# The last seven tiles' rows of the first layer made inside the first route; their logits from the squared relus

## The chip, the cores and the metric

The kernel runs on one core of a Trainium2 chip. The metric is the device time of the whole program in microseconds (us). The engines are TensorE (PE; its weight loads are listed as PEld), VectorE (DVE), ScalarE (ACT), GpSimd (POOL) and SyncE (SP), which here only issues DMAs.

## The reference, cut to what matters

Bucketed attention over 2 x 8 heads of 768 tokens gives `x` (1536 tokens, 512 columns). A dense layer follows, and then a second layer that sends each token to one of eight experts:

```python
def _moe_ref(x, w_in, w_out):
    h = np.maximum(x @ w_in, 0.0)
    return (h * h @ w_out).astype(np.float32)

def _moe2_ref(x, w_gate, w1, w2):
    logits = x @ w_gate
    order = np.argsort(-logits.flatten())
    # in this order a token takes an expert, if it has none and the expert
    # has fewer than N // E = 192 tokens
    ...
    for e in range(E):
        mask = assigned == e
        h = np.maximum(x[mask] @ w1[e], 0.0)
        out[mask] = h @ w2[e]
```

The assignment needs the logits of all 1536 tokens before the first expert can start.

## The kernel before

Three stages follow one another: attention, the first layer (`first_layer`), and `experts`, which also holds the routing.

**The first layer** takes the tokens in `CHUNKS` = 4 chunks of `HALF` = 384 tokens. For each chunk it goes through `FT` = 16 tiles of 128 hidden units. Products are made from 32-bit operands split in a high part (a rounded copy) and a low part (the rest). For a tile `f` of a chunk:

- PE, `hidden` (L946): 12 products of 384 columns into bank `PB[f % 2]`.
- ACT, `tile`: the relu out of the bank (L952), its square as high part `h_hi` (L954), then `in_high` (L963), the high part of the `w_in` tile two tiles on, and `out_high` (L966), that of the next `w_out` tile.
- DVE, `hidden`: the square in 32 bits (L1143) and its rest `h_lo` (L1146).
- POOL, `both_low`: the low parts of the `w_in` tile (L970) and of the `w_out` tile (L974). `hidden` two tiles on waits for the first (`wils`).
- PE, `rows` (L1227): 9 products of 512 columns (three token tiles by hi-hi, hi-lo, lo-hi), which add this tile's part to the 384 rows in banks `PB[2]` to `PB[4]`.

PE runs one tile ahead: `hidden(f + 1)`, then `rows(f)`. The order on each engine is the order of the code; semaphores join the engines. During the next chunk's first tiles, ACT copies the rows out, SP stores them to `y_rows` in DRAM, PE turns them (`turn`, L1241) and multiplies them with `w_gate` (`logits`, L1249). Behind the fourth chunk no tile is left to do this beside: ACT copies (L1135), PE turns (L1302) and multiplies (L1310), DVE and ACT copy between them, and a barrier between the two code blocks (L1864) ends the stage.

**The routing** finds which tokens an expert gets. `choose` (DVE, from L1537) takes each token's best expert; `route` goes through five digit levels (`LEVELS`). In each level DVE compares (L1561), PE counts with 12 products of 8 columns (L1719), DVE looks which experts fill (L1569), PE sums (L1721), DVE takes the digit. Then come three more steps (L1725; L1687 and L1688; L1694), the last of which makes the list of tokens. ACT copies the list (L1465), POOL gathers those rows from `y_rows` by an indirect DMA (L1427), PE turns them (L1741) and the expert starts (L1776, L1790). The later routes run between products of the experts; for the first there are none. `keep_warm` (L1799) issues idle products of 512 columns there, five behind each of its steps 10 and 11, and more in the steps of the second route.

SP loads the first half of the first expert's `w1` (L1409) when the route has named the expert.

## Time and profile before

| | us |
|---|---|
| median of 3 runs | 799.44 (798.57 to 799.66) |
| the profiled execution, its own time | 798.89 |
| its span, first to last instruction | 797.2 |
| PE busy | 771.8 (97%) |
| DVE busy | 368.7 (46%) |
| ACT busy | 378.6 (47%) |
| POOL busy | 400.0 (50%) |

The span is what the profile sees of the profiled execution; 1.69 us of its time lie outside. Busy time counts an engine's instructions; since the records of matmuls overlap, a stream's cost is read from start to start and not from the durations.

### The profile page before, as it was taken

How to read it: one execution, taken by the hardware profiler on the slowest of the kernel's cores; microseconds unless marked ns; L12 is line 12 of the kernel's file. 1: busy time of each engine (PE TensorE's matmuls, PEld its weight loads, DVE VectorE, ACT ScalarE, POOL GpSimd, SP SyncE). 2: the span in 40 equal slices, each digit the busy share in tenths (PEclk: the TensorE clock that was granted, in tenths of full speed). 3: DMA queues.
4: the chain of work that ended last, by engine and by line, in shares of the span. 5: the costliest groups of instructions: out<-in, count | busy, mean ns of one | idle time of the engine just before them, and what ended most of it. 6: DMA issues, size and time to landing. Idle time of an engine off the chain costs nothing. (4 is left out here: it accounts for less than half of the span.)

```text
span 797.2 us, 13826 instructions
## 1 busy us (share of the span) xinstructions
PE 771.8 (97%) x4620; PEld 700.2 (88%) x4622; DVE 368.7 (46%) x854; ACT 378.6 (47%) x664; POOL 400.0 (50%) x326
## 2 busy tenths in 40 slices
PE   7999999999999999999999999996799999999996
PEld 6898889889978888999999999995399999999996
DVE  7576576666754454232242225224654554454000
ACT  3677767767677655535555554552021222122221
POOL 5677777777686786656555666562100120011101
PEclk9999999999999999999999999998599999999999
DMA  7675776665554000000010001001264743654741
GB/s 161 145 175 134 154 163 161 144 160 133 128 114 137 0 1 0 14 28 0 0 39 0 0 0 41 0 0 40 74 230 161 249 148 133 224 190 164 263 136 40
DMA packets 44220, 81.44 MB, mean 102 GB/s; under 512 B 17192, under 2 KB 17192, under 8 KB 43664
## 3 DMA queue, kind: packets, MB, share of 16 engines
q1 hardware_dynamic: 41968, 74.58, 33.3%
q0 software_dynamic: 2048, 6.29, 2.4%
q8 instruction: 25, 0.41, 0.2%
q14 instruction: 19, 0.16, 0.1%
q10 hardware_dynamic: 160, 0.00, 0.0%
HBM read 54.55 MB, written 6.29 MB: 76 GB/s over the span
## 5 line engine op out<-in xcount | busy, mean ns | idle before, releaser
L312 POOL TENSOR_TENSOR pt_lo<-pt,pt_hi 128x768 fp32r<-128x768 f32 x64 | 117.8, 1846 | 51.2 <-ACT pt_hi L449 43.8
L946 PE MATMUL banks<-xt_hi,split_parts 128*128 128x384 f32 (+1 forms) x512 | 141.3, 337 | 0.5 <-POOL split_parts L970 0.5
L970 POOL TENSOR_TENSOR split_parts<-w_in_sb,split_parts 128x512 fp32r<-128x512 f32 x64 | 85.0, 1329 | 85.4 <-ACT split_parts L963 84.1
L1143 DVE TENSOR_TENSOR h<-relu 128x384 f32<-128x384 f32 x64 | 43.0, 671 | 177.2 <-ACT relu L952 177.1
L1227 PE MATMUL banks<-split_parts,h_hi 128*128 128x512 f32 x384 | 120.6, 395 | 0.2
L442 ACT ACTIVATE pt<-banks 128x768 f32<-128x768 f32 x96 | 78.1, 813 | 65.3 <-PE banks L719 55.0
L563 DVE TENSOR_REDUCE mx<-banks 128x1 f32<-128x768 f32 x96 | 90.5, 957 | 22.8 <-PE banks L747 18.7
L946 PEld LDWEIGHTS banks<-xt_hi,split_parts 128*128 128x128 f32 x512 | 93.5, 188 | 3.5 <-issue 0.9
L1776 PE MATMUL banks<-x_cols,w_in_sb 128*128 128x192 f32 x512 | 92.6, 333 | 0.4 <-ACT x_cols L1471 0.4
L1790 PE MATMUL banks<-expert_hidden,w_out_sb 128*128 128x192 f32 x512 | 92.2, 332 | 0.0
L974 POOL TENSOR_TENSOR split_parts<-w_out_sb,split_parts 128x512 fp32r<-128x512 f32 x64 | 84.5, 1320 | 13.7 <-ACT split_parts L966 13.7
L946 PE MATMUL banks<-xt_lo,split_parts 128*128 128x384 f32 (+1 forms) x256 | 86.1, 336 | 0.0
L1776 PEld LDWEIGHTS banks<-x_cols,w_in_sb 128*128 128x128 f32 x512 | 82.4, 191 | 2.4 <-issue 0.8
L1790 PEld LDWEIGHTS banks<-expert_hidden,w_out_sb 128*128 128x128 f32 x512 | 83.2, 191 | 0.6
L1227 PEld LDWEIGHTS banks<-split_parts,h_hi 128*128 128x128 f32 x384 | 70.4, 188 | 13.3 <-DVE h_lo L1146 1.4
L1434 POOL DMA_INDIRECT out<-expert_out,rows_of_out x14 | 13.2, 946 | 135.6 <-ACT expert_out L1486 133.5
L1227 PE MATMUL banks<-split_parts,h_lo 128*128 128x512 f32 x192 | 75.9, 395 | 0.0
L952 ACT ACTIVATE relu<-banks 128x384 f32<-128x384 f32 x64 | 31.5, 492 | 86.5 <-PE banks L946 86.5
L718 PE MATMUL banks<-qa,ka 128*128 128x384 f32 x190 | 68.7, 362 | 0.8 <-ACT pt L442 0.7
L719 PE MATMUL banks<-qb,kb 128*128 128x384 f32 x190 | 63.8, 336 | 0.0
L966 ACT ACTIVATE split_parts<-w_out_sb 128x512 fp32r (+1 forms) x64 | 40.6, 634 | 41.0 <-PE banks L1227 41.0
L1494 ACT ACTIVATE expert_hidden<-banks 128x192 f32<-128x192 f32 x64 | 21.2, 332 | 71.7 <-PE banks L1776 71.7
(239 smaller groups left out, 1329.8 us busy)
## 6 DMA issues: line engine op xcount, KB each, us to landing
w_out_sb<-in_moe_w SPq DMA_DIRECT2D x8, 2048.0 KB, 8.4
w_in_sb<-in_moe_w SPq DMA_DIRECT2D x7, 2048.0 KB
w_in_sb<-in_moe_w_in SPq DMA_DIRECT2D x8, 512.0 KB, 6.9
w_out_sb<-in_moe_w_out SPq DMA_DIRECT2D x8, 512.0 KB, 5.7
w_out_sb<-in_k SPq DMA_DIRECT2D x16, 192.0 KB, 3.9
w_out_sb<-in_q SPq DMA_DIRECT2D x16, 192.0 KB, 4.0
v_raw<-in_v SPq DMA_DIRECT2D x16, 192.0 KB, 3.7
ka<-split_parts SPq DMA_DIRECT2D x16, 192.0 KB, 3.0
```

Of the source, the lines that this page charges most:

```text
L312: pool.tensor_tensor(pt_lo[x % 2][:], pt[j % 2][:], pt_hi[x % 2][:].bitcast(fp32), ALU.subtract).then_inc(los, 1)
L442: act.activation(halves(pt[j % 2]), both(ST), ACT.Exp, scale=SCALE).then_inc(ex, 1)
L563: dve.tensor_reduce(mx[:, j:j + 1], both((PREP, SM)[j % 2]), AX.XY, ALU.max).then_inc(mxs, 1)
L718: pe.matmul(ST[:, h, 0:HALF], ka[i][:, kc], qa[i][:, c], start=True, stop=False)
L719: last = pe.matmul(ST[:, h, 0:HALF], kb[i][:, kc], qb[i][:, c], start=False, stop=True)
L946: last = pe.matmul(PB[i][:, 0:HALF], w_[:, k, :], x_[:, xs], start=n == 0, stop=n == 3 * DT - 1)
L970: pool.tensor_tensor(wil[i], in_view(f), wih[i].bitcast(fp32), ALU.subtract).then_inc(wils, 1)
L974: pool.tensor_tensor(wol[i], out_view(f), woh[i].bitcast(fp32), ALU.subtract).then_inc(wols, 1)
L1143: dve.tensor_tensor(h32[i][:], r32[i][:], r32[i][:], ALU.mult)
L1227: last = pe.matmul(PB[2 + t][:], h_[:, tc], w_[:], start=start and n == 0, stop=stop and n == 2, skip_group_check=True)
L1776: last = pe.matmul(PB[2 + f % 2][:, 0:CAP], w1s[i][:, k, f * P:(f + 1) * P], xgt[:, k, :], start=k == 0, stop=k == DT - 1)
L1790: last = pe.matmul(PB[4 + d % 2][:, 0:CAP], w2s[i][:, f, d * P:(d + 1) * P], hs[:, f, :], start=f == 0, stop=f == F2T - 1)
```

## The change

- The fourth chunk keeps its 16 `hidden` steps, but makes the `rows` products of its first `F0` = 9 tiles only. The squared relus of tiles 9 to 15 and the split parts of their `w_out` tiles are kept (`kept`, `late_parts`), most of them in space that the attention's result no longer needs. The `w_out` parts are made during the third chunk: on every second tile from tile 3 on ACT makes one high part more and POOL one low part more (7 each).
- The 63 products left out (3 token tiles x 7 hidden tiles x 3) go to `late_rows`: 6 behind the last `hidden`, 57 between the steps of the first route (`FILL`), where the ten `keep_warm` products go.
- The fourth chunk's logits are a sum of two. The rows of tiles 0 to 8 are copied out (`part`), turned (`part_turn`) and multiplied (`part_logits`, 16 columns wide, half of them zeros) beside the last `hidden` steps. For tiles 9 to 15 the logits come from the squared relus times `wogs`, which is `w_out` times `w_gate` in a high and a low part: `gate_sums_of`, two products of 384 columns for each of tiles 9 to 14, and `last_logits` for tile 15, which also turns those sums (3 products) and adds all up in `PB[6]`. It runs behind the barrier; DVE adds the halves by one reduction (L1868 of the new kernel).
- `w_out` times `w_gate` for the seven tiles is made by DVE during the first three chunks: 56 times `tensor_tensor_reduce` over 128x512 (three after a tile in chunk 0, two in chunks 1 and 2). SP loads the columns of `w_gate` as eight rows on all partitions (a further input `gate_rows`), and ACT copies each row to PSUM (8 copies), from where DVE reads it.
- DVE's square reads the relu's bank beside the relu (`scalar_tensor_tensor`) and no longer the relu twice. `hidden` of tile g waits for `h_lo` of tile g - 2 in place of its relu.
- The fourth chunk's rows are stored in three DMAs, each behind one ACT copy in `experts`; the DVE's wait for the stores in level 1 of the first route goes, POOL's wait before the first gather stays. On SP the three stores stand ahead of the load of `w1`.
- Constants of the routing (DVE, POOL) are made one or two a tile in the fourth chunk and not in one go.

The core of the diff:

```diff
+F0 = 9
+REST = FT - F0
+LATE_PARTS = {3: 9, 5: 10, 7: 11, 9: 12, 11: 13, 13: 14, 15: 15}
+PRODUCTS = 3 * CT * REST
+AHEAD = 6
+FILL = (14, 1, 6, 1, 5, 1, 5, 1, 5, 1, 4, 12, PRODUCTS)
...
+    def late_rows(pe, first, last):
+        for x in range(first, min(last, PRODUCTS)):
+            t, r = divmod(x, 3 * REST)
+            f, n = divmod(r, 3)
+            f += F0
...
+            h_, w_ = ((h_hi, w_hi), (h_hi, w_lo), (h_lo, w_hi))[n]
+            done = pe.matmul(PB[2 + t][:], h_[:, t * P:(t + 1) * P], w_, start=False, stop=r == 3 * REST - 1, skip_group_check=True)
+            if r == 3 * REST - 1:
+                done.then_inc(row_tile, 1)
...
         def _(dve):
-                dve.tensor_tensor(h32[i][:], r32[i][:], r32[i][:], ALU.mult)
+                dve.scalar_tensor_tensor(h32[i][:], PB[i][:, 0:HALF], 0.0, r32[i][:], ALU.max, ALU.mult)
...
+            def gate_part(c, x):
+                n, d = divmod(x, REST)
+                e = GATES * c + n
...
+                dve.tensor_tensor_reduce(made[:], wo[:, (F0 + d) * DM:(F0 + d + 1) * DM], PB[5 + n][:], 1.0, 0.0, ALU.mult, ALU.add,
+                                         wog[:, d, e:e + 1])
...
             def hidden(g, x0, i):
-                pe.wait_ge(relus, g - 1)
+                pe.wait_ge(hls, g - 1)
                 split["hidden"](pe, g, x0, i)
...
+            def gate_sums_of(f):
...
+                pe.wait_ge(hls, last_g + f + 1)
+                for n, h_ in enumerate(kept(f)):
+                    last = pe.matmul(PB[7][0:2 * E, P:P + HALF], wogs[:, f - F0, :], h_, start=f == F0 and n == 0, stop=f == FT - 2 and n == 1)
...
+            def last_chunk(x0):
+                c = CHUNKS - 1
+                for f in range(FT):
+                    g, i = last_g + f, f % 2
+                    if f + 1 < FT:
+                        hidden(g + 1, x0, 1 - i)
+                    else:
+                        late_rows(pe, 0, AHEAD)
...
+                    elif f == F0 + 1:
+                        part_turn(0)
+                    elif f == F0 + 2:
+                        part_turn(1)
+                    elif f == F0 + 3:
+                        part_logits(0)
+                        part_turn(2)
+                    elif f == F0 + 4:
+                        part_logits(1)
+                    elif f == F0 + 5:
+                        part_logits(2)
+                    if f < F0:
+                        rows(g, i, f == 0, False)
+                    elif f < FT - 1:
+                        gate_sums_of(f)
...
         def _(sp):
+            for t in range(CT):
+                sp.wait_ge(y_tile, t + 1)
+                at = (CHUNKS - 1) * HALF + t * P
+                sp.dma_start(y_rows[at:at + P, :], last_rows[t]).then_inc(stored, 16)
...
-            pool.wait_ge(stored, 16 * CHUNKS)
             pool.memset(oh[:, CH:P], 0.0).then_inc(padded, 1)
+            pool.wait_ge(stored, STORED)
...
-                    if l == 1 and not past(s, 1):
-                        dve.wait_ge(stored, 16 * CHUNKS)
...
+            dve.wait_ge(logit, 1)
+            dve.tensor_reduce(L[:, NT - CT:NT, :], PB[6][:, 0:2 * E * CT].rearrange("p (t a e) -> p t e a", t=CT, a=2), AX.X, ALU.add)
...
-            for k in range(STEPS):
+            last_logits(pe).then_inc(logit, 1)
+            at = AHEAD
+            for k, fill in enumerate(FILL):
+                late_rows(pe, at, at + fill)
+                at += fill
                 routing(0, k)
-                if 2 * NL <= k < STEPS - 1:
+                if k >= 2 * NL and at >= PRODUCTS and k < STEPS - 1:
                     keep_warm(5)
```

**PE in the fourth chunk, around one of its later tiles.** Before, a tile's `rows` (L1227) stand behind each `hidden` (L946):

```order
L946 MATMUL banks0<-xt_lo,split_parts 128x384
L946 MATMUL banks0<-xt_hi,split_parts 128x384
L1227 MATMUL banks1<-split_parts,h_hi1 128x512 x2
L1227 MATMUL banks1<-split_parts,h_lo1 128x512
L1227 MATMUL banks1<-split_parts,h_hi1 128x512 x2
L1227 MATMUL banks1<-split_parts,h_lo1 128x512
L1227 MATMUL banks2<-split_parts,h_hi1 128x512 x2
L1227 MATMUL banks2<-split_parts,h_lo1 128x512
```

Now (L958 is `hidden`, L1401 `part_logits`, L1392 `part_turn`, L1410 `gate_sums_of`), between `hidden` of tile 13 and of tile 14:

```order
L958 MATMUL banks0<-xt_hi,split_parts 128x384 x2
L958 MATMUL banks0<-xt_lo,split_parts 128x384
L958 MATMUL banks0<-xt_hi,split_parts 128x384
L1401 MATMUL banks3<-w_gate_and_zeros,y_t0 128x16 x4
L1392 MATMUL banks2<-ident,turned 128x128 x4
L1410 MATMUL banks3<-xt_hi,gate_of_hidden_parts 16x384
L1410 MATMUL banks3<-xt_lo,gate_of_hidden_parts 16x384
L958 MATMUL banks0<-xt_hi,split_parts 128x384
```

The nine products of 512 columns have gone from here; two of 384 columns and the small ones of the logits have come.

**PE from the last hidden tile to the first route.** Before: the last rows, the turned rows (L1302), the logits (L1310), the two blocks' branches, and the route's counting:

```order
L1227 MATMUL banks2<-split_parts,h_hi1 128x512 x2
L1227 MATMUL banks2<-split_parts,h_lo1 128x512
L1302 MATMUL banks2<-ident,y_rows_sb 128x128 x4
L1302 MATMUL banks3<-ident,y_rows_sb 128x128 x4
L1302 MATMUL banks0<-ident,y_rows_sb 128x128 x4
L1310 MATMUL banks3<-w_gate_sb,y_t0 128x8 x4
L1310 MATMUL banks3<-w_gate_sb,y_t1 128x8 x4
L1310 MATMUL banks3<-w_gate_sb,y_t2 128x8 x4
L1864 UNCONDITIONAL_BRANCH
L1683 UNCONDITIONAL_BRANCH
L1719 MATMUL banks3<-chosen16,reaches 128x8 x12
L1721 MATMUL banks3<-fills,level_weights 128x8
```

Now: the last `gate_sums_of`, six late products (L1026), the branches, and `last_logits` (L1498, L1503):

```order
L1410 MATMUL banks3<-h_hi0,gate_of_hidden_parts 16x384
L1410 MATMUL banks3<-h_lo0,gate_of_hidden_parts 16x384
L1026 MATMUL banks1<-xt_hi 128x512
L1026 MATMUL banks1<-xt_lo,xt_hi 128x512
L1026 MATMUL banks1<-xt_hi,xt_lo 128x512
L1026 MATMUL banks1<-xt_hi 128x512
L1026 MATMUL banks1<-xt_lo,xt_hi 128x512
L1026 MATMUL banks1<-xt_hi,xt_lo 128x512
L2070 UNCONDITIONAL_BRANCH
L1882 UNCONDITIONAL_BRANCH
L1498 MATMUL banks3<-ident,relu0 128x16 x3
L1503 MATMUL banks3<-gate_of_hidden_parts,h_hi1 128x16
```

Turns and logits of the rows stand ahead of the barrier, in the run of hidden tiles; what is left behind the branches is `last_logits` and the late products after it.

**PE in the digit levels of the first route.** Before, nothing stands between its steps until L1799:

```order
L1719 MATMUL banks3<-chosen16,reaches 128x8 x12
L1721 MATMUL banks3<-fills,level_weights 128x8
L1719 MATMUL banks3<-chosen16,reaches 128x8 x12
L1721 MATMUL banks3<-fills,level_weights 128x8
L1725 MATMUL banks3<-chosen_counts,ones16 128x192
L1799 MATMUL banks1<-level_table0,level_weights 128x512 x5
L1687 MATMUL banks3<-members_up_to_tile,ones16 128x24
```

Now, two levels (L1918 counts, L1920 sums, L1026 are late products):

```order
L1918 MATMUL banks3<-chosen16,reaches 128x8 x12
L1026 MATMUL banks1<-xt_hi 128x512
L1920 MATMUL banks3<-fills,level_weights 128x8
L1026 MATMUL banks1<-xt_lo,xt_hi 128x512
L1026 MATMUL banks1<-xt_hi,xt_lo 128x512
L1026 MATMUL banks1<-xt_hi 128x512
L1026 MATMUL banks1<-xt_lo,xt_hi 128x512
L1026 MATMUL banks1<-xt_hi,xt_lo 128x512
L1918 MATMUL banks3<-chosen16,reaches 128x8 x12
L1026 MATMUL banks1<-xt_hi 128x512
L1920 MATMUL banks3<-fills,level_weights 128x8
```

Each counting step has five products of 512 columns ahead of it, each summing step one.

**DVE in the first three chunks.** Before, a tile is its two operations:

```order
L1143 TENSOR_TENSOR h0<-relu0 128x384
L1146 TENSOR_TENSOR h_lo0<-h0,h_hi0 128x384
L1142 REGISTER_ALU
L1143 TENSOR_TENSOR h1<-relu1 128x384
L1146 TENSOR_TENSOR h_lo1<-h1,h_hi1 128x384
```

Now, in chunk 1 (L1262 is the new reduction, with a short second instruction for its sum):

```order
L1246 SCALAR_TENSOR_TENSOR h0<-banks0,relu0 128x384
L1249 TENSOR_TENSOR h_lo0<-h0,h_hi0 128x384
L1262 ISA gate_products,gate_of_hidden<-w_out_sb,banks3 128x512
L1262 ISA gate_of_hidden 128x1
L1262 ISA gate_products,gate_of_hidden<-w_out_sb,banks3 128x512
L1262 ISA gate_of_hidden 128x1
L1246 SCALAR_TENSOR_TENSOR h1<-banks0,relu1 128x384
L1249 TENSOR_TENSOR h_lo1<-h1,h_hi1 128x384
```

Two reductions that read PSUM stand behind each tile's pair.

## Rows read from the trace of the kernel before

**Rows 1.** Page, part 2, 40 equal slices of the span: granted TensorE clock in tenths

```profile
PEclk9999999999999999999999999998599999999999
```

**Rows 2.** Windows: stretch, length, busy us of each engine (xinstructions), clock, DMA, GB/s

```profile
541.00:550.00 9.00, 8.22 (x54) 7.03 (x52) 2.93 (x6) 3.41 (x6) 2.78 (x14) 1.00 0.23 87
550.00:572.00 22.00, 10.96 (x90) 6.77 (x92) 14.35 (x67) 0.00 (x0) 0.14 (x1) 0.50 0.13 42
572.00:580.00 8.00, 7.63 (x49) 3.57 (x48) 4.67 (x16) 1.04 (x3) 2.06 (x2) 0.66 0.28 76
580.00:797.00 217.00, 210.63 (x1612) 205.93 (x1612) 81.92 (x354) 47.89 (x140) 28.48 (x30) 1.00 0.51 178
```

**Rows 3.** Timeline, PE, 536-550: start us, us from first start to last end, instruction

```profile
536.61 0.63 PE L1227 MATMUL banks<-split_parts,h_hi 128*128 128x512 f32 x2
...
538.69 0.34 PE L946 MATMUL banks<-xt_hi,split_parts 128*128 128x384 f32 x1
...
540.78 0.63 PE L1227 MATMUL banks<-split_parts,h_hi 128*128 128x512 f32 x2
...
545.00 1.50 PE L1302 MATMUL banks<-ident,y_rows_sb 128*128 128x128 f32 x12
546.38 2.85 PE L1310 MATMUL banks<-w_gate_sb,y_t 128*128 128x8 f32 x24
```

**Rows 4.** Timeline, DVE, first operation of the routing

```profile
549.75 0.25 DVE L1537 TENSOR_REDUCE best<-logits 128x12 f32<-128x96 f32 x1 [0.31 <-PEq L1864]
```

**Rows 5.** Timeline, one tile of a steady chunk, ACT, DVE and POOL

```profile
503.54 0.49 ACT L952 ACTIVATE relu<-banks 128x384 f32<-128x384 f32 x1 [1.41 <-PE banks L946]
...
504.06 0.56 DVE L1143 TENSOR_TENSOR h<-relu 128x384 f32<-128x384 f32 x1 [2.97 <-ACT relu L952]
...
504.69 0.56 DVE L1146 TENSOR_TENSOR h_lo<-h,h_hi 128x384 fp32r<-128x384 f32 x1
...
505.36 1.29 POOL L970 TENSOR_TENSOR split_parts<-w_in_sb,split_parts 128x512 fp32r<-128x512 f32 x1 [1.70 <-ACT split_parts L963]
```

**Rows 6.** Timeline, DVE and POOL at the start of the last chunk

```profile
479.29 0.93 DVE L1143 TENSOR_TENSOR h<-relu 128x384 f32<-128x384 f32 x1 [2.97 <-ACT relu L952]
...
481.33 1.61 POOL L970 TENSOR_TENSOR split_parts<-w_in_sb,split_parts 128x512 fp32r<-128x512 f32 x1
...
481.71 1.28 DVE L1151 COPY y_t<-banks 128x512 f32<-128x512 f32 x2
```

**Rows 7.** Waits, PEld, 270-545: who waited <- for whom: us in total, times, longest

```profile
PEld banks L1227 <- DVE h_lo L1146: 1.4, 4, 0.5
```

**Rows 8.** Timeline, PE, parts of the first route

```profile
552.62 1.02 PE L1719 MATMUL banks<-chosen,reaches 128*128 128x8 f16 x12 [3.40 <-DVE reaches L1561]
...
561.25 0.19 PE L1721 MATMUL banks<-fills,level_weights 128*128 128x8 bf16 x1 [0.25 <-DVE fills L1569]
562.44 0.86 PE L1719 MATMUL banks<-chosen,reaches 128*128 128x8 f16 x12 [1.00 <-DVE reaches L1561]
...
564.92 0.34 PE L1725 MATMUL banks<-chosen_counts,ones 128*128 128x192 f16 x1 [1.17 <-DVEq L1583]
...
568.28 0.20 PE L1687 MATMUL banks<-members_up_to_tile,ones 128*128 128x24 f16 x1 [0.89 <-DVEq L1616]
...
571.94 2.72 PE L1799 MATMUL banks<-level_table,level_weights 128*128 128x512 bf16 x6
```

**Rows 9.** Timeline, SP, ACT and POOL around the copies of rows and the first gather

```profile
543.88 1.91 ACT L1135 ACTIVATE y_rows_sb<-banks 128x512 f32<-128x512 f32 x3 [1.79 <-PE banks L1227]
...
567.97 0.41 SPq L1409 DMA_DIRECT2D w_in_sb<-in_moe_w  x1
...
572.12 0.17 ACT L1465 ACTIVATE token_list<-banks 96x4 int32<-96x4 f32 x1 [25.45 <-PE banks L1694]
...
573.28 1.13 POOL L1427 DMA_INDIRECT x_rows<-y_rows,token_list  x1 [23.13 <-ACT token_list L1465]
```

**Rows 10.** DMA issues, 545-551: KB each, median us from issue to landing

```profile
y_rows<-y_rows_sb SPq DMA_DIRECT2D x1, 768.0 KB, 3.5
```

353 lines of the change are left out of this document (242 added, 111 removed).

## The prediction

> **What bounds the kernel now.** I read the windows by stage first, then PE's timeline where a stage ends, then the waits. From 580 us on PE is busy 210.63 of 217 us at full clock [rows 2]; the first layer before 541 is the same stream of products without gaps: `hidden` starts every 4.17 us, 2.08 us of `rows` (536.61 to 538.69) and 2.09 us of `hidden` (538.69 to 540.78) [rows 3]. Between them lies the one stretch where PE is not the bound: 550 to 572 us, PE busy 10.96 of 22 us, DVE 14.35, and the clock at 0.50, which is 1.2 GHz; the page shows the same dip in slices 28 and 29 [rows 1, 2]. That is the first route: a chain DVE, PE, DVE, PE, in which PE's gaps are about 1.0 us ahead of each counting step and 0.25 us ahead of each summing step [rows 8]. Ahead of it stands a second serial piece: after the last rows at 545.00 come the turns (to 546.38), the logits (2.85 us), DVE's copy and the barrier, so that `choose` starts at 549.75 [rows 3, 4]. Everything after the first gather hangs on the moment when the route has a token list. So the question is how much earlier `choose` starts, and whether the route grows.
>
> **The path up to `choose`, taken away.** Seven tiles' `rows`: 7 x 2.08 = 14.6 us [rows 3]. The tail from 545.00 to 549.75: 4.75 us [rows 3, 4]. Sum 19.3 us.
>
> **The same path, added.** Gate sums: 12 products of 384 columns; `hidden` makes 12 in 2.09 us, so 2.09 us. Turns: 12, as before, 1.38 us (545.00 to 546.38). `part_logits`: 12 products of 32-bit data, 24 records, as before 2.85 us (8 columns then, 16 now; 0.119 us a record is far more than 16 columns take in a stream of 384 in 0.174 us, so width costs nothing). Six late products at 2.08 / 9 = 0.231 us: 1.39 us. Then the last product's end (0.17 us) and the barrier: before, PE ended at 549.23 and DVE went on at 549.75, so 0.5 us [rows 3, 4]. `last_logits`: 9 products, three of 32-bit data, 12 records at 0.119 us plus 0.1: 1.53 us. DVE's reduction instead of a copy: 0.35 us, by the 0.25 us of `best` [rows 4] with its release. So far 10.3 us.
>
> **Stalls in the run of hidden tiles.** `hidden(f + 2)` needs the low part from POOL. From a tile's relu (503.54) to that part (505.36 + 1.29 = 506.65) it is 3.1 us, so 3.2 us from the end of `hidden(f)` [rows 5]. `rows` used to cover this: PE came back after 4.17 us. Now PE has `hidden(f + 1)`, gate sums (0.35 us) and a turn (0.46 us) or logits (0.95 us): 2.9 to 3.4 us. The two are equal within 0.3 us, so most tiles wait little or nothing. ACT has 0.64 us more per tile for three of them (a third of 1.91 us) [rows 9] and fits: it was idle 1.41 us ahead of a relu [rows 5] and has no `out_high` there any more. One stall I expect: DVE's `columns` copy (0.64 us) [rows 6] pushes tile 11's square and `h_lo` into POOL's operation; `h` then takes 0.93 us for 0.56 us and POOL 1.61 us for 1.29 us [rows 5, 6]. I take 0.5 us in all; the bounds are 0 and 2.5 us (0.4 us for each of six tiles). Total added 10.8 us: `choose` starts **8.5 us earlier**.
>
> On that contention the Trainium skill, "SBUF — State Buffer", section "SBUF: two separate sides", says that a DVE operation with two SBUF inputs and a GpSimd operation that reads SBUF take one port pair as an exclusive lock, the later one waiting for the other's whole instruction. The trace agrees in kind [rows 6]; by the full rule `h_lo` of tile 11 would wait out POOL's 1.29 us and the gate sums behind it about 0.4 us, which is inside the 0.5 us above.
>
> **The first route.** It took 549.75 to 572.29 (end of the list copy) [rows 4, 9]. The fills must fit its gaps at full clock: five products are 1.16 us; from a summing step (561.25) to the next counting step (562.44) are 1.19 us [rows 8]. One product of 0.231 us stands in the gap of 0.25 us. Fourteen products are 3.2 us, and `choose` to the first counting step (552.62) 2.9 us, but six of the 12 counts wait for DVE's second half anyway. Twelve products are 2.8 us, from 564.92 to 568.28 are 3.4 us. So they fit, with a tenth here and there: cost 0 to 1.5 us over 13 places. Against it stands the clock: with PE fed, the 12 counts (0.86 to 1.02 us) and the sums go at full clock, 0.02 to 0.1 us less each over five levels. I take -0.3 us, with bounds -0.6 and +1.5 us.
>
> **Store and gather.** The third row tile's last product now stands just ahead of the token list: issued behind the step at 568.28, in new time 568.3 - 8.8 = 559.5, done 559.8; ACT copies 0.64 us, SP issues at 560.5. The store before took 3.5 us for 768 KB [rows 10]; this one is 256 KB. Bounds 1.2 us (a third) and 3.5 us; I take 3.0 us, near the upper one, since a DMA's start and end do not shrink with its size: landed 563.5. The token list is copied by 572.29 - 8.8 = 563.5 [rows 9]. The two meet; the gather is late by 0 to 0.5 us. SP can load `w1` only behind that store: at about 562 instead of 559.2 (567.97 - 8.8). That is still 2.5 us ahead of the gather's own start at 564.5 (573.28 - 8.8), and the expert needs the gather and its turns first, so I cost it at nothing; without that cover it would be up to 2.8 us. I take +0.3 us.
>
> The Trainium skill, "DMA: Bandwidth & Descriptors", section "Anatomy of one DMA — SWDGE (gpsimd) path", puts one DMA at 2.0 us plus bytes at 436 GB/s, an estimate of 2.6 us here; by it the gather would not be late at all and the sum 0.3 us better. No row shows a 256 KB store.
>
> **Chunks 0 to 2.** DVE: up to three reductions of 128x512 a tile. Nearest row: a copy of 128x512 out of PSUM, 0.64 us; with its second instruction I take 0.75 us. DVE is idle 2.97 us a tile [rows 5], 3 x 0.75 = 2.25 us fit; two in chunks 1 and 2 fit easily. They would cost from 0.99 us each on. ACT's 15 further copies (0.64 us) have 1.4 us idle ahead of each relu. POOL's seven more (1.3 us) have 1.70 us idle and stand on every second tile. SP's three loads of gate rows stand ahead of its stores, in microseconds in which nothing waits for SP. All this hides behind PE. A small gain: `h` no longer reads SBUF twice, so it stops colliding with POOL; PE waited 1.4 us in four places for `h_lo` [rows 7]. I take -0.4 us, bounds -1.4 and +0.5 us. The wait on `h_lo` in place of the relu costs nothing, since `rows` of that tile, ahead of it, waited for it already; in the late run `h_lo` is there 2.0 us after `hidden`, before the low part (3.2 us).
>
> **Sum.** -8.5 - 0.3 - 0.4 + 0.3 = -8.9 us. Against the profiled execution's 798.89 us that is 790.0 us; it is 0.55 us under the median of 799.44 us, against which it is 790.5 us. I forecast **790.2 us**, between the two.
>
> **Rivals.**
> - **The hidden run is bound by its loop** over ACT, DVE and POOL: every tile waits 0.4 us or more because the three collide. Six tiles, +2.4 us: 792.6 us. For it: PE's cover is within 0.3 us of the loop. Against: two of six tiles have half a microsecond more cover.
> - **The fills are late or the store is.** The products of 512 columns sit in PE's queue when DVE answers: +0.1 to 0.2 us at 13 places, or the gather waits 1.5 us more: 792 us.
> - **The clock stays down, and it is slower.** If PE still fell to 1.2 GHz at the barrier, a fill would take 2.72 / 6 = 0.45 us [rows 8]. Then a level has 5 x 0.45 + 0.45 us of fills for gaps of 1.25 us: +1.3 us x 5; the first fill 14 x 0.45 = 6.3 us for 2.9 us, +3.4 us; the twelve 5.4 us for 3.4 us, +2 us. Together about +12 us: 802 us. It decides from about 0.35 us a fill on. Before the fall PE's clock was 1.00 through turns and logits [rows 2] and fell with PE idle from 549.23 to 552.6; now the longest idle piece is the barrier's 0.5 us. So it is unlikely.
> - **The reductions hold POOL up.** If a reduction with one operand in PSUM collided with POOL as `h` does, or took 1.3 us or more, DVE's tile would be 1.2 + 3 x 1.3 = 5.1 us in chunk 0, +0.9 us over seven tiles, and up to that in chunks 1 and 2: +6 to +20 us, 796 to 810 us. Against it: two PSUM copies beside POOL ran in 1.28 us [rows 6].
> - **It does not shorten the path**: the late products only move, if the route were bound by PE. Its 50% busy share [rows 2] excludes that.
>
> **How the numbers follow.** Forecast 0.63; hidden run 0.14; fills or store 0.11; clock 0.05; reductions 0.05; nothing gained 0.02. The first three are faster, of the reductions a fifth: 0.89. The range takes in the first three with the bounds of their costs (all good ends -2 us, the run's bad end and the store together +5 us): 788.0 to 795.0 us. Within 0.2% (1.6 us, about what a measurement of this kernel can tell from no change): 0.03. Slower: 0.08.
>
> **What the new profile would show.** PE's last hidden tile ends near 536 us instead of 541; the route's first operation starts near 541.2; the granted clock stays 1.00 through the route; gaps ahead of the steps vanish while a level stays 2.3 us long; the first gather starts near 564.5; PE's waits in chunks 0 to 2 stay under 1 us; the reductions take 0.7 to 0.8 us. It would be wrong with a clock of 0.50 there, reductions over 1 us, or a gather that waits for the store by over a microsecond.

## The result, and the profile after the change

| | kernel before | changed kernel |
|---|---|---|
| median of the executions | 799.55 us (798.57 to 799.66, 4) | 790.27 us (789.38 to 791.75, 4) |
| profiled execution, and its span | 798.89 us, 797.2 us | 790.34 us, 788.6 us |
| mean granted TensorE clock of that execution | 0.982 | 0.992 |
| ratio of the times, 95% interval | | 0.9888 (0.9871 to 0.9906) |

The changed kernel takes 1.1% less, 9.3 us of the medians and 8.55 us between the two profiled executions. The forecast was 790.2 us. Line numbers below are the changed kernel's: `hidden` is L958, `rows` L1358, the late row products L1026, the gate sums L1410, turns and logits of the late run L1392 and L1401, the last logits L1498 and L1503, the reductions of w_out times w_gate L1262, the route's steps L1918 to L1893, the filler products that nothing reads L1998, the turns of the gathered rows L1940, the first expert's products L1975.

The windows by stage answer to [rows 2] (columns as there: length, busy time of PE, PEld, DVE, ACT, POOL, granted clock, DMA share, GB/s):

```profile
531.00:540.00 9.00, 8.70 (x59) 7.85 (x58) 2.72 (x8) 2.51 (x5) 0.66 (x2) 1.00 0.00 1
540.00:561.00 21.00, 18.92 (x124) 13.52 (x122) 13.58 (x63) 1.79 (x3) 0.00 (x0) 1.00 0.08 28
561.00:562.00 1.00, 0.59 (x10) 0.60 (x11) 0.81 (x4) 0.00 (x0) 0.00 (x0) 0.62 0.58 217
562.00:571.00 9.00, 9.00 (x53) 4.59 (x53) 4.88 (x18) 1.04 (x3) 2.05 (x2) 0.50 0.63 208
571.00:572.00 1.00, 1.00 (x10) 0.96 (x10) 0.11 (x1) 0.00 (x0) 0.00 (x0) 0.76 1.07 416
572.00:789.00 217.00, 209.89 (x1606) 205.10 (x1605) 81.50 (x353) 47.75 (x140) 28.47 (x30) 0.99 0.50 174
```

Before, PE was busy for 10.96 of the 22 us of the first route, at 1.2 GHz; now it is busy for 18.92 of 21 us, at full clock. That is the row work in the waits. But the clock still falls to 1.2 GHz, 11 us later than before: it is down from about 561.2 to 571.5 us, and from 562 on PE has no idle time there. The forecast did not have that stretch.

The timeline of PE and DVE at the end of the first layer, changed kernel (start, duration, instruction):

```profile
534.99 0.96 PE L1401 MATMUL banks<-w_gate_and_zeros,y_t 128*128 128x16 f32 x8
...
535.80 0.34 PE L1410 MATMUL banks<-h_hi,gate_of_hidden_parts 128*16 128x384 f32 x1
535.97 0.34 PE L1410 MATMUL banks<-h_lo,gate_of_hidden_parts 128*16 128x384 f32 x1
536.15 0.39 PE L1026 MATMUL banks<-xt_hi 128*128 128x512 f32 x1
...
537.30 0.40 PE L1026 MATMUL banks<-xt_hi,xt_lo 128*128 128x512 f32 x1
...
538.00 0.81 PE L1498 MATMUL banks<-ident,relu 16*128 16x16 f32 x6 [0.30 <-PEq L2070]
...
539.61 0.21 DVE L1868 TENSOR_REDUCE logits<-banks 128x24 f32<-128x48 f32 x1 [2.64 <-PE banks L1503]
...
539.89 0.25 DVE L1736 TENSOR_REDUCE best<-logits 128x12 f32<-128x96 f32 x1
```

The first operation of `choose` starts at 539.89, 9.86 us before its old place [rows 4]. The rest of the way, changed kernel, the timeline of PE, DVE, ACT, SP and POOL:

```profile
542.76 1.01 PE L1918 MATMUL banks<-chosen,reaches 128*128 128x8 f16 x12
...
543.80 0.17 DVE L1765 TENSOR_TENSOR fills<-banks,capacity_left 128x8 bf16<-128x8 f32 x1 [0.62 <-PE banks L1918]
...
558.85 0.19 PE L1886 MATMUL banks<-members_up_to_tile,ones 128*128 128x24 f16 x1 [0.31 <-DVEq L1812]
...
560.05 0.32 SPq L1600 DMA_DIRECT2D y_rows<-turned  x1
...
561.41 0.88 PE L1893 MATMUL banks<-ids_by_column,row_onehot 128*128 128x4 f16 x12 [2.02 <-DVEq L1842]
...
562.32 0.17 ACT L1661 ACTIVATE token_list<-banks 96x4 int32<-96x4 f32 x1 [2.30 <-PE banks L1893]
...
563.42 1.13 POOL L1623 DMA_INDIRECT x_rows<-y_rows,token_list  x1 [25.04 <-ACT token_list L1661]
...
568.40 1.52 PE L1940 MATMUL banks<-ident,x_rows 96*128 96x96 f32 x8
...
571.02 0.77 PE L1975 MATMUL banks<-x_cols,w_in_sb 128*128 128x192 f32 x2
```

The first gather is issued 9.86 us earlier too (563.42 for 573.28 [rows 9]); PE idles for 2.02 us ahead of the last step of the route, and at the end of that the clock falls. The turns L1940, eight of them, take 1.52 us at 1.2 GHz. In the kernel before, five filler products stand ahead of the route's last step, and PE idles for 0.57 us (its timeline of PE):

```profile
571.22 0.86 PE L1694 MATMUL banks<-ids_by_column,row_onehot 128*128 128x4 f16 x12 [0.57 <-DVEq L1646]
```

The changed kernel issues these fillers only once all 63 row products are out, and one row product is left for the last step.

The costliest groups of DVE, changed kernel (busy time in all, mean ns of one, idle time ahead):

```profile
L1262 DVE CUSTOM_DVE_ANT_0 gate_products<-w_out_sb,banks 128x512 f32<-128x512 f32 x56 | 38.3, 684 | 3.9 <-issue 0.5
L1249 DVE TENSOR_TENSOR h_lo<-h,h_hi 128x384 fp32r<-128x384 f32 x59 | 36.6, 620 | 4.4
L1246 DVE SCALAR_TENSOR_TENSOR h<-banks,relu 128x384 f32<-128x384 f32 x64 | 35.7, 557 | 134.9 <-ACT relu L964 134.9
L1262 DVE DVE_READ_ACCUMULATOR2_ANT gate_of_hidden<- 128x1 f32 x56 | 4.6, 82 | 0.0
```

A reduction costs DVE 684 + 82 = 766 ns, and 56 of them, 43 us of DVE in three chunks, lie beside PE without one wait for a low part. The square, with its factor from PSUM, takes 557 ns in the mean.

The first chunk even became shorter. The relu that closes its sixteenth step of `hidden` and `rows`, counted from 274.00 before and from 274.78 after, in the timeline of ACT, before and after:

```profile
342.54 0.49 ACT L952 ACTIVATE relu<-banks 128x384 f32<-128x384 f32 x1 [2.40 <-PE banks L946]
```

```profile
342.33 0.49 ACT L964 ACTIVATE relu<-banks 128x384 f32<-128x384 f32 x1 [2.39 <-PE banks L958]
```

68.54 us became 67.55 us. In this execution the chunk began 0.8 us later, so 0.2 us came through. That start scatters: it lies from 274.08 to 274.91 us in the eight traced executions whose code up to there is the changed kernel's, and from 273.99 to 274.54 in three of the kernel before. So a distance within the chunk says more than the time of day at its end.

### The profile page after: what moved, and what is told of

Read it like the earlier page. It is cut to its first block and busy times, and to the rows that moved or that the text cites. A ratio compares the mean times of both kernels' runs of the same rounds, so it can differ in the third digit from the quotient of the medians.

```text
span 788.6 us, 13550 instructions
## 1 busy us (share of the span) xinstructions
PE 772.6 (98%) x4636; PEld 701.7 (89%) x4636; DVE 394.9 (50%) x971; ACT 382.9 (49%) x675; POOL 398.6 (51%) x326
## 5 line engine op out<-in xcount | busy, mean ns | idle before, releaser
L958 PE MATMUL banks<-xt_hi,split_parts 128*128 128x384 f32 (+1 forms) x512 | 141.3, 337 | 0.2 <-POOL split_parts L982 0.2
L1358 PE MATMUL banks<-split_parts,h_hi 128*128 128x512 f32 x342 | 107.1, 394 | 0.0
L1246 DVE SCALAR_TENSOR_TENSOR h<-banks,relu 128x384 f32<-128x384 f32 x64 | 35.7, 557 | 134.9 <-ACT relu L964 134.9
L958 PEld LDWEIGHTS banks<-xt_hi,split_parts 128*128 128x128 f32 x512 | 93.5, 188 | 3.6 <-issue 0.9
L1975 PE MATMUL banks<-x_cols,w_in_sb 128*128 128x192 f32 x512 | 92.8, 333 | 0.0
L958 PE MATMUL banks<-xt_lo,split_parts 128*128 128x384 f32 (+1 forms) x256 | 86.1, 336 | 0.0
L1975 PEld LDWEIGHTS banks<-x_cols,w_in_sb 128*128 128x128 f32 x512 | 82.6, 191 | 2.2 <-issue 0.6
L986 POOL TENSOR_TENSOR split_parts<-w_out_sb,split_parts 128x512 fp32r<-128x512 f32 x57 | 74.0, 1298 | 10.4 <-ACT split_parts L978 10.4
L1358 PEld LDWEIGHTS banks<-split_parts,h_hi 128*128 128x128 f32 x342 | 62.9, 188 | 10.5
L1358 PE MATMUL banks<-split_parts,h_lo 128*128 128x512 f32 x171 | 67.6, 395 | 0.0
L461 ACT ACTIVATE pt_hi<-pt 128x768 fp32r<-128x768 f32 x64 | 54.2, 846 | 1.7
```

Source lines behind the costliest of these rows:

```text
L461: act.activation(pt_hi[x % 2][:], pt[j % 2][:], ACT.Copy).then_inc(his, 1)
L958: last = pe.matmul(PB[i][:, 0:HALF], w_[:, k, :], x_[:, xs], start=n == 0, stop=n == 3 * DT - 1)
L986: pool.tensor_tensor(wol[i], out_view(f), woh[i].bitcast(fp32), ALU.subtract).then_inc(wols, 1)
L1358: last = pe.matmul(PB[2 + t][:], h_[:, tc], w_[:], start=start and n == 0, stop=stop and n == 2, skip_group_check=True)
L1975: last = pe.matmul(PB[2 + f % 2][:, 0:CAP], w1s[i][:, k, f * P:(f + 1) * P], xgt[:, k, :], start=k == 0, stop=k == DT - 1)
```

## The experiments

**The main term: what the late row products cost in the open.** All 63 stand ahead of the last logits.

```
-AHEAD = 6
+AHEAD = PRODUCTS
-FILL = (14, 1, 6, 1, 5, 1, 5, 1, 5, 1, 4, 12, PRODUCTS)
+FILL = (0,) * STEPS
```

> One part of the change undone by position: all 63 late row products stand ahead of the last logits and the first choose, not 6 of them, and none in the waits of the first route; the logits still come from squared relus times w_out w_gate. Theory (the rows' price is what they occupy of TensorE where nothing hides them): 57 products more at 0.23 us put the choose 13.1 us later, at about 553.0 instead of 539.9; the route between is as long as before, and TensorE idles in it, so its clock falls there and is back before the first expert, which gives 0.7 to 2 back: time 789.3 + 13.1 - 1 = 801.4 (800 to 803). Rival (half of the gain is from the logits coming without their rows, not from the place of the row products): the choose is only 6 to 8 us later, time 796 to 798. Second rival (the rows in the waits lengthened the route by waits of their own, so taking them out shortens it by 1 us or more): 799 to 800.

Measured: 801.86 us (801.53 to 805.61, 7 executions), 1.0038 (1.0018 to 1.0059) of the kernel before. Its timeline of DVE at the choose, and its windows:

```profile
552.72 0.25 DVE L1736 TENSOR_REDUCE best<-logits 128x12 f32<-128x96 f32 x1
```

```profile
557.00:579.00 22.00, 14.23 (x100) 7.52 (x100) 14.15 (x64) 0.17 (x1) 2.06 (x2) 0.50 0.17 57
```

The choose is 12.8 us later, and this execution entered the first layer 0.3 us earlier; so 57 products took 13.1 us, 0.231 us each, and the first theory holds to half a microsecond. (Since all row products are out here, the ten filler products behind steps 10 and 11 are issued again.) With the logits by the new way but the rows in the open, the kernel is slower than before. So the whole gain is in the place of the rows: the identity only makes the logits independent of them.

**The same kernel again, for its spread.** Nothing is edited.

> The changed kernel again, beside the others on one chip. All theories: 790.3 us, 9.2 us under the kernel before. In its profile the granted clock of TensorE is 1.00 up to about 561 us and 0.50 from there to about 571 us. If the fall is an accident of one run it is absent here; if it comes from the 2.0 us in which TensorE waits ahead of the token list, it is here again.

Measured: 789.32 us (788.31 to 792.07, 5 executions), ratio 0.9879 (0.9864 to 0.9894). The two executions above 791 us have a mean clock of 0.990, the other three 0.995 or 0.996. The profiled one is of the longer ones, 791.9 us; its windows:

```profile
562.00:563.00 1.00, 1.00 (x5) 0.34 (x3) 0.85 (x5) 0.00 (x0) 0.16 (x1) 0.68 0.94 154
563.00:576.00 13.00, 12.44 (x71) 9.01 (x70) 4.81 (x14) 1.20 (x3) 1.89 (x2) 0.50 0.77 254
```

Here the stretch at 1.2 GHz lasts until 576, over the first expert's first 16 products. From the start of the first to the start of the counting step behind the sixteenth they take 5.93 us (570.45 to 576.38), where the execution above took 3.77 us (571.02 to 574.79). So the changed kernel has a spread of 3.8 us, where the kernel before beside it had 1.3 us (798.65 to 799.94, 11 executions), and in these two traces the difference is where this stretch ends. The executions with a mean clock of 0.995 or 0.996 have no trace. A kernel below has 0.998 or 0.999 without any low stretch, so theirs lasted 3 to 5 us by an estimate (0.002 to 0.003 of 788 us, at half the clock).

**Filler products ahead of the route's last step only.**

```
             for k, fill in enumerate(FILL):
...
+                if k == STEPS - 1:
+                    keep_warm(8)
                 routing(0, k)
```

> The changed kernel with eight idle products of 512 columns (1.7 us at full clock) in the 2.0 us gap ahead of the token list. Theory, the gap brings the clock down and the low clock costs the turns ahead of the first expert: clock 1.00 throughout, the first expert product 0.6 to 1.0 us earlier against the token list than in the changed kernel, time 0.7 to 1.1 us less. Rival, the clock falls for another reason (the many products of 8 columns) or is harmless there: time within 0.3 us of the changed kernel.

Measured: 791.44 us (789.58 to 792.94, 5), ratio 0.9895 (0.9881 to 0.991). The theory's clock and time did not come. The gap ahead of L1893 went from 2.02 to 0.28 us, and the clock still fell, 4 us later; the timeline and the windows:

```profile
563.94 0.86 PE L1918 MATMUL banks<-chosen,reaches 128*128 128x8 f16 x12 [1.11 <-DVE reaches L1763]
```

```profile
566.00:576.00 10.00, 9.30 (x52) 7.92 (x53) 3.04 (x9) 1.20 (x3) 0.00 (x0) 0.50 0.75 253
```

At full clock the fillers of the second route are over sooner, which opens a gap of 1.11 us there. The fall was moved, and all of the expert's first 16 products lie in the low stretch: 6.03 us (570.22 to 576.25), as in the longer execution above. The interval of the ratio overlaps that of the changed kernel, so the times do not show that the new place is dearer.

**The kernel before, with fillers in its first route.** They stand where the changed kernel has its row products, and ahead of the last step.

```
-            for k in range(STEPS):
+            for k, fill in enumerate((12, 1, 6, 1, 5, 1, 5, 1, 5, 1, 4, 12, 9)):
+                keep_warm(fill)
                 routing(0, k)
-                if 2 * NL <= k < STEPS - 1:
-                    keep_warm(5)
```

> The kernel before with idle products of 512 columns in all gaps of its first route (12, 1, 6, 1, 5, 1, 5, 1, 5, 1, 4, 12, 9 ahead of the thirteen steps), nothing else changed. Theory, the gain of the change is the shorter way to the first operation of the routing and the route itself is a chain of latencies: the route takes 22.3 to 22.9 us as before (22.5), and only the turns and first products of the expert gain: 0.3 to 1.2 us less than before. Rival, most of the 9 us came from TensorE at full clock in the first route: 4 us less or more.

Measured: 803.27 us (798.98 to 804.86, 6), ratio 1.0047 (1.0032 to 1.0063). The median is slower, with more clock. The profiled execution had the clock at 1.00 throughout and took 798.98 us, 0.4 us less than the kernel before beside it (799.34 us), as the theory had it; so it showed no cause for the other five. Its windows in the waits of the second route:

```profile
572.00:580.00 8.00, 5.69 (x50) 3.31 (x49) 4.63 (x16) 1.03 (x3) 2.06 (x2) 1.00 0.28 73
```

A second look:

> The kernel before with filler products in the waits of its first route, once more, for the place of the clock's fall: six executions of it took 798.98 to 804.86, and the one whose trace is shown, 798.98, had no fall at all. Theory (where the second route's waits leave TensorE idle for 0.3 to 1.1 us at a time, the clock falls behind them, and then ten microseconds and more of the first experts run at 1.2 GHz): time 803 to 805, the granted clock is 1.00 up to about 575 and 0.50 in a stretch of 10 us or more that reaches behind 585, in which TensorE has no idle time. Rival (the filler products themselves take time or clock somewhere before the route's end, in the attention or the route's own steps): the choose or the first expert starts 2 us or more later than at 549.75 and 580.08, at a full clock.

Measured: 803.32 us, one execution, with these windows:

```profile
577.00:578.00 1.00, 0.75 (x3) 0.30 (x4) 0.57 (x3) 0.00 (x0) 0.26 (x1) 0.65 0.43 148
578.00:587.00 9.00, 9.00 (x51) 6.88 (x50) 3.20 (x9) 1.20 (x3) 0.00 (x0) 0.50 0.77 254
```

The theory holds for the later part. PE was busy 1.02 of 2 us at 574 to 576, in the waits of the second route, and then about 10 us at 1.2 GHz came, half of them in the first expert. But the clock had not been 1.00 up to there. It had already fallen once, behind the barrier, and was back at about 553.4; the timeline of PE:

```profile
550.71 3.87 PE L1799 MATMUL banks<-level_table,level_weights 128*128 128x512 bf16 x11 [0.92 <-PEq L1863]
```

These eleven fillers took 2.54 us in the execution at full clock. The first counting step came 1.8 us later than there, 0.6 us of it by a later choose. Of the 4.3 us between the two executions 2.3 us are there when the first expert starts (582.41 for 580.15), so what the rival expected of the expert's start came too, though at a low clock; 2.2 us come in the expert's first 16 products. And the gaps alone do not decide: the execution at full clock has the same ones (1.10 and 0.73 us, PE busy for 5.69 of 8 us), and its clock did not fall. What decides between the two no run shows.

In the kernel before [rows 2] the low stretch began at 550, lay in the route, where PE has idle time to lose, and was over before the expert.

**No gap left between the first route and the first expert.** If a low stretch costs what of it lies in the expert, taking all gaps away must help.

```
+                if k == STEPS - 1:
+                    keep_warm(8)
                 routing(0, k)
...
-            for k, fill in enumerate((6, 1, 4)):
+            for k, fill in enumerate((10, 2, 6)):
...
-            keep_warm(3, PB[2])
+            keep_warm(4, PB[2])
```

> The changed kernel with more filler products that nothing reads: 8 ahead of the last step of the first route, and 10, 2, 6 and 4 where the second route has 6, 1, 4 and 3, so that TensorE has no gap over 0.5 us between the first route and the first expert. Theory (the granted clock falls after a stretch in which TensorE idled and stays down for 10 to 14 us, and what that costs is what of the stretch lies in the first expert): the clock stays at 2.4 GHz from 540 to the first expert at about 570.3 and through it; the first expert's first 16 products with the route's step beside them take 3.8 us and not 5.9, span 786.0 to 787.0, time 787.5 to 788.8, clock 0.998. Rival (the clock falls later whatever is done, as for a budget that is used up): a stretch of 10 us at 1.2 GHz stands somewhere behind 566 with TensorE busy in it, 3 to 5 us are lost: time 790.5 to 793.

Measured: 788.85 us (788.69 to 789.41, 4), ratio 0.9866 (0.9849 to 0.9882). The windows:

```profile
560.00:571.00 11.00, 10.01 (x81) 5.74 (x80) 6.75 (x25) 1.15 (x4) 2.05 (x2) 1.00 0.57 180
571.00:580.00 9.00, 9.00 (x79) 8.76 (x78) 3.44 (x15) 1.57 (x5) 0.00 (x0) 1.00 0.85 321
```

The clock is 1.00 through the expert, 0.998 or 0.999 in the mean of all four, and the spread is 0.7 us where it was 3.8 us. The same 16 products with their counting steps take 3.54 us (570.38 to 573.92). The budget rival falls. The median gains 0.5 us on that of the changed kernel (789.32), which is within the intervals; what the run shows is that the longer executions are gone, which were 3 us above.

**One part undone: the square reads the relu twice from SBUF.**

```
-                dve.scalar_tensor_tensor(h32[i][:], PB[i][:, 0:HALF], 0.0, r32[i][:], ALU.max, ALU.mult)
+                dve.tensor_tensor(h32[i][:], r32[i][:], r32[i][:], ALU.mult)
```

> Only one part of the change is undone: VectorE again squares the relu from SBUF twice (it reads r32 with r32) and no longer takes the first factor from PSUM. Theory (the change's PSUM operand only keeps VectorE and GpSimd apart and was hidden work): the square's mean goes back from 557 ns to about 670 ns over its 64 instructions and the low part's from 620 to about 680, 0.2 us a product in sum, and TensorE loses at most the 0.2 us a chunk by which the relus came earlier: time 789.3 to 790.3, the relu that starts the third chunk at 474.5 instead of 474.3. Rival (the reductions of the change live on the VectorE time that the PSUM operand freed): with 56 reductions of 0.77 us as well, the low parts come late, TensorE's weight loads wait for them again (1.4 us and more a chunk), and the time is 793 or more.

Measured: 793.73 us (790.37 to 794.17, 4), ratio 0.9913 (0.989 to 0.9937). The group of the square, and the relu that closes the first chunk's sixteenth step:

```profile
L1246 DVE TENSOR_TENSOR h<-relu 128x384 f32<-128x384 f32 x64 | 48.1, 752 | 115.4 <-ACT relu L964 115.1
```

```profile
343.44 0.49 ACT L964 ACTIVATE relu<-banks 128x384 f32<-128x384 f32 x1 [2.39 <-PE banks L958]
```

752 ns, not the 670 of my theory, and the first chunk takes 68.53 us again, as long as before the change. Three of its steps slip by 0.3 to 0.4 us. PE's own list of waits has nothing there, but that of its weight loads has, in the same three steps (PEld, 270 to 545 us):

```profile
PEld banks L1358 <- DVE h_lo L1249: 1.1, 3, 0.5
```

So the low parts do come late, as in the kernel before [rows 7]: that is the rival's way, though in the first chunk alone. The choose starts at 541.33, 1.44 us later: 1.0 us by the first chunk, 0.3 us by the first step of the fourth, 0.1 us by a later start. The other 2 to 3 us are the clock: here it fell at 568 and came back at about 578.5, and some 6 us of that lie in the expert, which starts at 572.39. The rival's time (793 us or more) came, but only in part for its reason; the one execution with a mean clock of 0.996 took 790.37 us.

**One part undone: the gate's row read from SBUF.**

```
-                dve.tensor_tensor_reduce(made[:], wo[:, (F0 + d) * DM:(F0 + d + 1) * DM], PB[5 + n][:], 1.0, 0.0, ALU.mult, ALU.add,
+                dve.tensor_tensor_reduce(made[:], wo[:, (F0 + d) * DM:(F0 + d + 1) * DM], gate[:, n, :], 1.0, 0.0, ALU.mult, ALU.add,
...
+            sp.wait_ge(hls, FT + 1)
...
+            sp.wait_ge(hls, 2 * FT + 1)
```

> Only one part of the change is undone: the reductions that make w_out times w_gate read the gate's row from its SBUF buffer, not from the copy in PSUM, and the two later loads of that buffer wait until the reductions of their stage are through. Theory: the reduction reads two SBUF operands, holds 684 ns no longer but about 1 us while GpSimd works on its own product (GpSimd's 1.30 us grows to 1.6 us where they meet), and nothing waits: time 789.3 to 790.3. Rival: with some 56 times 0.3 us more VectorE time, 17 us over the three chunks, and GpSimd's split later, TensorE waits for weights or low parts in each chunk: relu of the third chunk at 476 or later, time 791 to 795.

Measured: 798.38 us (795.61 to 800.09, 10), ratio 0.9982 (0.997 to 0.9994). Nearly the whole gain is gone, and the time lies above the rival's range too. The group and the wait:

```profile
L1264 DVE CUSTOM_DVE_ANT_0 gate_products<-w_out_sb,gate_rows_sb 128x512 f32<-128x512 f32 x56 | 65.4, 1167 | 3.9 <-issue 0.5
```

```profile
PE banks L1360 <- DVE h_lo L1251: 4.7, 9, 1.1
```

The timelines of DVE and of POOL in the first chunk:

```profile
327.95 0.69 DVE L1264 CUSTOM_DVE_ANT_0 gate_products<-w_out_sb,gate_rows_sb 128x512 f32<-128x512 f32 x1
...
328.76 1.60 DVE L1264 CUSTOM_DVE_ANT_0 gate_products<-w_out_sb,gate_rows_sb 128x512 f32<-128x512 f32 x1
```

```profile
328.52 1.29 POOL L982 TENSOR_TENSOR split_parts<-w_in_sb,split_parts 128x512 fp32r<-128x512 f32 x1 [1.71 <-ACT split_parts L975]
```

Alone the reduction takes 0.69 us. The one that starts 0.24 us behind POOL's operation takes 1.60 us: it waits for POOL's end (329.81) and then does its 0.69 us, give or take 0.14. The rival holds, by DVE: its idle time ahead of the reductions is 3.9 us as in the changed kernel, so the later loads of the buffer made no part of it. The first chunk is 4.7 us longer, the third 2.2 us, and the choose starts at 546.68, 6.8 us later. The profiled execution (796.18 us, mean clock 0.996) is 5.8 us above the profiled one of the changed kernel; the six executions at 0.990 to 0.992 took 798.3 to 800.1 us, so the rest of the median goes with a lower clock.

PE idles for 2.02 us ahead of the route's last step here as well, up to 568.20, and the clock falls behind it; but it is back after 3.4 us. The windows of PE alone (length, busy time, clock, DMA share, GB/s):

```profile
568.00:569.00 1.00, 0.81 (x13) 0.91 0.34 127
...
572.00:573.00 1.00, 0.97 (x11) 0.88 1.04 410
```

The Trainium skill, "SBUF — State Buffer", section "SBUF: two separate sides", says that a DVE operation with two SBUF inputs and a GpSimd operation that reads SBUF exclude each other for the whole instruction of the first. The trace agrees with it in these rows, in length as well as in kind.

**The other chain: the third row tile's store.** Eight row products are moved from ahead of the route's last step but one to ahead of its last.

```
-FILL = (14, 1, 6, 1, 5, 1, 5, 1, 5, 1, 4, 12, PRODUCTS)
+FILL = (14, 1, 6, 1, 5, 1, 5, 1, 5, 1, 4, 4, PRODUCTS)
```

> The changed kernel with eight of the late products moved from ahead of step 11 to behind it, so that the third row tile is ready 1.9 us later and its store too; TensorE is fed up to the token list as in the run with idle products there. Theory, the store lands just before the gather could start (562.05 against 562.5 us): the gather is late by about 1.4 us against the token list, and the clock stays at 1.00, so the time is 0.3 to 1.0 us above the changed kernel and 1.2 to 1.6 above the one with idle products. Rival, the store has slack of 2 us or more: the same time as with the idle products.

Measured: 795.09 us (793.23 to 795.69, 5), ratio 0.9945 (0.9932 to 0.9957). POOL and PE:

```profile
564.48 1.13 POOL L1623 DMA_INDIRECT x_rows<-y_rows,token_list  x1 [26.48 <-DMA y_rows<-turned]
...
569.40 1.54 PE L1940 MATMUL banks<-ident,x_rows 96*128 96x96 f32 x8 [1.26 <-DMA x_rows<-y_rows,token_list]
```

Now the gather waits for the store, where in the changed kernel it waits for the token list. It starts 2.36 us behind the end of the list's copy (562.12), where it starts 0.93 us behind it in the changed kernel: 1.4 us late, as the theory had it. The turns are 1.6 us later than in the changed kernel's second look (567.81). The clock did not stay at 1.00: it was low from 567 to 577, over an expert that starts at 572.04. Against the execution of that second look, whose low stretch lies over the expert as well (791.9 us), the profiled one (793.36 us) is longer by 1.5 us, which is the gather. The median is 5.8 us above that of the second look; its executions have no trace.

**Row products moved to where they fit better**, with the fillers of the kernel that holds the clock.

```
-FILL = (14, 1, 6, 1, 5, 1, 5, 1, 5, 1, 4, 12, PRODUCTS)
+FILL = (14, 1, 6, 1, 4, 1, 4, 1, 5, 1, 5, 13, PRODUCTS)
```

> The kernel with more filler products, and beside that one late row product fewer in front of the counting steps of levels three and four and one more in front of the two last steps. Theory (in those levels VectorE waits 0.80 us for a counting step and 0.62 in the others, because a row product stands in front of the step): the gaps of VectorE there fall to 0.65, the first expert starts 0.25 us earlier: 788.6. Rival (the counting steps wait for VectorE's comparison, and the products ahead of them end in time): no change, 788.85, with gaps as before. Worse rival: the products moved to the last steps make the store late by 0.23 us: 789.1.

Measured: 788.51 us (788.02 to 789.0, 4), ratio 0.9859 (0.9842 to 0.9875), the shortest of all. The fourth level's gap on DVE in this kernel:

```profile
550.74 0.16 DVE L1765 TENSOR_TENSOR fills<-banks,capacity_left 64x8 bf16<-64x8 f32 x1 [0.69 <-PE banks L1918]
```

It was 0.80 us (0.81 in the changed kernel). From the choose to the expert it is 30.19 us (539.52 to 569.71), where it was 30.35 us (540.03 to 570.38), so 0.16 us of the 0.25 expected came. The 0.34 us between the medians are within the intervals.

**Three row products fewer ahead of the last logits.**

```
-AHEAD = 6
+AHEAD = 3
...
-                    keep_warm(8)
+                    keep_warm(5)
```

> As the kernel with filler products and the row products moved, and three late row products ahead of the last logits where there were six; the other three follow the last counting step, in place of three filler products. Theory (the barrier ahead of the last logits is reached by TensorE last, 0.6 us behind VectorE's last low part at 537.10, so row products ahead of it cost their full 0.23 us each): the choose starts 0.6 us earlier (at most 0.69) at 539.4, the store of the third row tile is issued as before, and the time is 788.0. Rival (what ends last at the barrier is VectorE's low part or another engine): the choose is earlier by 0.2 us or less, time 788.5. Worse rival (the third row tile's store is late for the gather): x_rows land later than the route's step that needs them, and the turns wait 0.3 us or more for them: time 788.9 or more.

Measured: 790.07 us (788.12 to 790.61, 4), ratio 0.9874 (0.9857 to 0.9892). DVE, POOL and PE:

```profile
538.95 0.25 DVE L1736 TENSOR_REDUCE best<-logits 128x12 f32<-128x96 f32 x1
...
562.57 1.13 POOL L1623 DMA_INDIRECT x_rows<-y_rows,token_list  x1 [25.14 <-DMA y_rows<-turned]
...
568.79 0.88 PE L1940 MATMUL banks<-ident,x_rows 96*128 96x96 f32 x8 [1.37 <-DMA x_rows<-y_rows,token_list]
```

The choose did come 0.57 us earlier than in the last kernel (0.69 us against its own last low part), as the theory said: products ahead of the barrier cost their full time. And the turns wait, as the worse rival has it, but the store has the small part in that. The gather is issued 0.3 us later than the token list would let it (1.20 us behind the list's end for 0.93), at 562.57, which is still 0.26 us earlier than in the last kernel. Its rows then took 4.6 us from issue to landing, where they took 3.7 (the DMA issues of this run, 555 to 575 us):

```profile
x_rows<-y_rows,token_list POOLq DMA_INDIRECT x2, 4.6
```

PE waits 1.37 us for them, and the turns start 1.0 us later than in the last kernel. Why they took longer no run shows; the load of `w_in` is under way beside them in both kernels. The interval of the ratio overlaps the last kernel's, and one of the four executions took 788.12 us.

## Why the forecast came out right, step by step

The time is within 0.1 us of the forecast, but that closeness is luck, because two errors cancel: the choose came 1.0 us earlier than forecast, and 1.3 us were lost between the gather and the end, most of it by a low clock. The path, the hidden work and the direction were right.

- **Path taken away.** 14.6 us of rows at 0.231 us a product: with the rows in the open, 57 products took 13.1 us, 0.231 us each. Right.
- **Path added.** Twelve turns took 1.1 us from start to start, but the gate sum behind each took 0.26 us where the others took 0.17; together that is the forecast's 1.38. 24 logits records 3 x 0.81 = 2.43 us, for 2.85, so in a stream of other products a record is shorter (0.101 us) than it was behind turns alone (0.119 us). The barrier took 0.30 us for 0.5. The other gate sums, late products and the last logits were as forecast. The stalls: one of 0.2 us, for 0.5; `hidden` of tile 12 starts at 523.01, 0.15 us behind the end of its low part on POOL. With 0.1 us less for DVE's reduction that is 1.0 of the 1.1 us by which this stretch beat the forecast; 0.28 us more stood at its start: the choose is 9.86 us earlier, for 8.5 + 0.4.
- **Collisions in the hidden run.** They happen, POOL's operation takes 1.66 us twice there where it took 1.29 us alone, and `hidden` starts 0.3 us or more behind their ends, so they cost nothing. The one stall is behind an operation of 1.29 us: that is the loop. The rival of a loop-bound run had 0.4 us in each of six tiles; one paid, half of that.
- **The route.** 22.60 us from choose to the end of the list copy, where it took 22.54 before; forecast -0.3 us. A full clock gained nothing there: in levels three and four DVE waited 0.81 us for a counting step that had one row product too many ahead of it, and moving these gave back 0.16 us.
- **Store and gather.** The third tile's 256 KB landed 2.0 us after its issue; I had taken 3.0 us, near the upper bound. So the gather waited for the token list alone, at +0.0 for +0.3 us. A gather starts 0.93 us behind the later of the two, here and, within 0.01 us, in the two kernels where it waits for the store. The store landed at 562.05 and the list's copy ended at 562.49, so the spare time was 0.4 us. With the store 1.9 us later against the list the gather was 1.4 us late. The Trainium skill's "DMA: Bandwidth & Descriptors", section "Anatomy of one DMA — SWDGE (gpsimd) path", has a fit that gives 2.6 us for 256 KB (an estimate: the fit is for GpSimd's path, and this is SP's queue); the 2.0 us measured are under it.
- **The clock: the step that failed.** I read the clock only for the first route and said the longest idle piece would be the barrier's 0.5 us. It was 2.02 us, ahead of the route's last step, where five filler products had stood. I had not asked what becomes of that place once the row products are used up, nor where the low stretch would lie. In the kernel before it lay from 550 to 576 and cost next to nothing: with fillers in its route and the clock at 1.00 throughout it took 0.4 us less. In the profiled execution of the changed kernel it lies from 561.2 to 571.5, in the other traced one from 562.4 to 576. From gather to expert 0.8 us were lost (the turns at 568.40 are 9.77 us ahead of before, the expert at 571.02 only 9.06 us), and 0.5 us more by the end. The kernel without a low stretch lost 0.1 of the 0.8 and 0.2 of the 0.5, so the clock's part is about 1.0 us here and about 3 us in the longer executions. The rival "the clock stays down" had the mechanism but for the wrong stretch, at 12 us.
- **Chunks 0 to 2.** Reductions 0.766 us, for 0.75; no wait for a low part. The gain is 1.0 us within the first chunk, for 0.4 in all; with a start 0.8 us later in this execution, -0.28 us are left. With the square read from SBUF the 1.0 us are gone, so it is the square's PSUM operand that made them. The two rows that this rested on were the right ones, and how much rested on them the forecast did not say. It gave a chance of 0.05 to reductions that collide with POOL. The gate's row in SBUF makes just that, and takes 6.8 us of the choose's 9.86 and 8 us of the median's 9. The PSUM operand of the reductions is the condition of the whole change.

Left open: why the low stretch lasts 10 us in one execution and 14 in another of one kernel, and 3.4 us in the kernel with the gate's row in SBUF, behind the same gap of 2.02 us; and why the same gaps are followed by a fall in one execution and not in another. No run told these apart.

## What to carry to other kernels

Work that fills the waits of a serial route is worth its full time on the path it leaves, so count that first. Then ask two things of the same trace: which operands the hidden work on DVE shares with POOL, since one operand in PSUM or two in SBUF decided 8 us here, and where TensorE's idle time will now lie, since a gap of one to two microseconds just ahead of a stretch that TensorE bounds can cost more than a long one far from it. A few products that nothing reads, in every such gap, kept the mean clock at 0.998 or 0.999 in all eight executions of two kernels; in one gap alone they only moved the fall.
